# Router stage of a fused attention and expert kernel: TensorE filler work replaced, overflow inversion moved behind the transposes, second gather released earlier

## The chip, the cores and the metric

The kernel runs on one core of one Trainium2 chip. The metric is the device time of one execution in microseconds (us), lower is better. Three executions of the kernel before took 742.91, 743.01 and 746.74 us; the median is 743.01 us.

## The reference, cut to what matters

Three stages follow each other. All numbers are float32.

```python
# 1. attention with exponential gates: batch 2, 8 heads, 768 positions, head size 40
#    per position: decay state C and n, add v x k, y = sigmoid(o) * (C q) / max(|n q|, 1)
x = attn_out as rows                      # N = 1536 rows of 320

# 2. mixture of 8 experts, 320 -> 1024 -> 320, each row goes to its two best
noisy = x @ w_gate + log1p(exp(x @ w_noise)) * noise
top2  = two largest of noisy;  top2_w = softmax over the two
for e in range(8):
    for k in range(2):
        mask = top2[:, k] == e
        out[mask] += top2_w[mask, k, None] * (relu(x[mask] @ w1[e]) @ w2[e])

# 3. four experts, every row goes to all, weighted by normalised domain_probs
for e in range(4):
    out += p[:, e:e+1] * (relu(x @ w1b[e]) @ w2b[e])
```

## The kernel before, in words

The program is written out by hand, one instruction stream for each engine (`block.tensor`, `block.vector`, `block.scalar`, `block.gpsimd`, `block.sync`), and the streams meet only at semaphores (`wait_ge`). An engine works through its stream in order. Five stretches follow each other: attention (to about 90 us), the router (to about 124 us), the hand-over of the first tiles (to about 135 us), expert layer 1 (to about 361 us) and expert layer 2 (to the end). The change lies in the router's end and in the hand-over.

**Router.** DVE finds for each of the 24 pairs of choice and row tile (`2 * NT`) where its rows go. For every pair it writes `in_row` (L793) and `ids` (L794) and counts up `rt_place`. TensorE turns these lists round: 24 small bf16 matmuls (L1099), in six groups of four (`INV = 4`), accumulate into the bank `psI` (in the trace `psF`). DVE then writes the row numbers `rowid` (L798) and counts up `rt_rows`. With them GpSimd starts indirect DMAs (`gather`, L462): one fetches 128 rows of 320 numbers from DRAM into a part of `xrows`; four make one visit. The function `gather(v)` waits before visit 1 until the first hidden product of visit 0 is done (`h_mm[0]`), and from visit 2 on until the transposes of the visit that used the same buffer are done (`tr_mm[0]`).

**Filler.** `idle_work(n)` (L1091) issues n matmuls 128x512 whose result nobody reads. They stand in five places: three ahead of each group of the router's inversion but the first (15 in all), one each into two further banks and 16 more behind the last group, two ahead of tiles 1, 2 and 3 in the hand-over (6), and three at its end. All read the first weights of expert 0, which is why `wh_done[0]` is waited for ahead of them.

**Hand-over.** As each of the four tiles of visit 0 lands (`xin_first[tt]`), TensorE transposes it with four matmuls against the identity (L1109 to L1111), ScalarE copies the result rounded to fp32r (`x_hi`, L601, and `x_end`, L603), and DVE writes the rest (`x_lo`, L885, `x_end`, L887). Ahead of the filler and transposes of tile 3, TensorE waits for `over_picked` (set behind L831) and runs a second inversion of 24 small matmuls (L1192) into `psO` (in the trace `psL`) for the slots that hold an expert's overflow. DVE needs it at L890, once it has done tile 3's part, to make the row numbers of the overflow slots (`over_rows`) and the positions of results (`rt_dest`).

**Layer 1.** A loop of 8 visits, one expert and up to 512 rows each (`visit1`). TensorE reads two flags (`value_load`) and branches to a form of a visit with four tiles or with three (384 columns, taken by visit 0). A visit has 8 steps: `up` is eight matmuls into `pH` (L1132 to L1139), `down` is three matmuls a tile into `pY` (L1147 to L1149). Step s + 1's `up` is issued ahead of step s's `down`, which waits for DVE's `h_lo` (L848). During steps 4 to 6 the tiles of the next visit are transposed out of the other `xrows` buffer. SyncE loads the weights of the next expert as the pieces of the staging buffers come free.

Data products are split in a high and a low part, so each logical product is three matmuls.

## Time and profile before

| | |
|---|---|
| median of 3 runs | 743.01 us (742.91 to 746.74) |
| the profiled execution: its own time | 742.91 us |
| its span, first to last instruction | 741.0 us |
| mean granted TensorE clock | 0.972 of full |
| TensorE busy | 684.0 us (92%), 4064 matmuls |
| weight loads (beside the matmuls) | 612.5 us (83%) |
| DVE busy | 399.3 us (54%) |
| ScalarE busy | 287.0 us (39%) |
| GpSimd busy | 102.0 us (14%) |
| filler L1091 | 42 matmuls, 116.6 to 134.3 us |

Times in the rows are counted from the first instruction of the span. PE is TensorE's matmuls, PEld its weight loads, DVE VectorE, ACT ScalarE, POOL GpSimd, SP SyncE. The granted clock is a share of 2.4 GHz: 1.00 is 2.4 GHz and 0.50 is 1.2 GHz. A matmul's duration in the rows is its time through a pipeline; in a chain of them the distance between two starts is what one costs. The profiled execution's own time is 1.91 us longer than its span, and 0.10 us under the median.

### The profile page before, as it was taken

The numbers are of one execution on the slowest core, as the hardware profiler recorded it, in microseconds if no ns is written. First come the engines' busy times: TensorE is split into PE (matmuls) and PEld (weight loads), VectorE is DVE, ScalarE is ACT, GpSimd is POOL, SyncE is SP. The second block draws the span as 40 slices with busy tenths as digits, with TensorE's granted clock in tenths as the row PEclk, the third lists the DMA queues.
The fourth block names the chain that finished last, engine by engine and source line by source line (L and its number), as shares of the span: only waits on it lengthen the run. The fifth ranks groups of instructions, "written<-read, shape, count | busy, mean of one in ns | idle before, by whom it ended". The sixth has DMA issues, their size and how long they took to land.

```text
span 741.0 us, 11122 instructions
## 1 busy us (share of the span) xinstructions
PE 684.0 (92%) x4064; PEld 612.5 (83%) x4065; DVE 399.3 (54%) x667; ACT 287.0 (39%) x470; POOL 102.0 (14%) x137
## 2 busy tenths in 40 slices
PE   2999967899999999999469999999999999999997
PEld 2888824799889899899458998998898898988886
DVE  7667668656536456455155545545554554454422
ACT  6644530454434454454123324333343342332311
POOL 5343302431020220200140100201200001000000
PEclk9999887999999999999869999999999999999999
DMA  8566693375535455340175333343442333422000
GB/s 206 148 148 155 190 367 96 100 213 165 152 128 164 112 169 171 109 136 17 58 222 168 100 102 118 103 128 110 117 131 82 101 95 124 128 85 73 0 0 35
DMA packets 32566, 93.12 MB, mean 126 GB/s; under 512 B 4848, under 2 KB 14832, under 8 KB 32528
## 3 DMA queue, kind: packets, MB, share of 16 engines
q1 hardware_dynamic: 25040, 76.23, 35.5%
q0 software_dynamic: 3264, 11.15, 5.3%
q10 hardware_dynamic: 4224, 5.24, 1.9%
q8 instruction: 24, 0.39, 0.2%
q14 instruction: 14, 0.11, 0.1%
HBM read 79.49 MB, written 13.11 MB: 125 GB/s over the span
## 4 chain that ended last, share of the span: by engine, by line
PE 88%; DVE 5%; issue 2%; DMA 1%; POOL 1%; ACT 1%; DVEq 0%; ACTq 0%; POOLq 0%
PE pY L1147 12%; PE pY L1149 12%; PE pY L1148 12%; PE pH L1132 9%; PE pH L1133 9%; PE pH L1134 9%; PE pH L1139 5%; PE pH L1137 5%; PE psS L976 3%; PE psYa L1029 3%; PE pT L1109 2%; PE psYa L1042 1%; PE psF L1063 1%; PE pH L1091 1%; PE psD L986 1%
## 5 line engine op out<-in xcount | busy, mean ns | idle before, releaser
L576 ACT ACTIVATE h_hi<-pH 128x512 fp32r<-128x512 f32 x160 | 95.7, 598 | 290.1 <-PE pH L1139 290.1
L848 DVE SCALAR_TENSOR_TENSOR h_lo<-pH,h_hi 128x512 fp32r<-128x512 f32 x160 | 110.5, 691 | 174.1 <-ACT h_hi L576 173.0
L1147 PE MATMUL pY<-w_hi,h_hi 128*128 128x320 f32 x608 | 189.2, 311 | 3.9 <-DVE h_lo L848 3.3
L1149 PE MATMUL pY<-w_hi,h_lo 128*128 128x320 f32 x608 | 187.8, 309 | 0.0
L1148 PE MATMUL pY<-w_lo,h_hi 128*128 128x320 f32 x608 | 187.7, 309 | 0.0
L1132 PE MATMUL pH<-x_hi,w_hi 128*128 128x512 f32 (+2 forms) x324 | 126.9, 392 | 6.1 <-issue 3.6
L1147 PEld LDWEIGHTS pY<-w_hi,h_hi 128*128 128x128 f32 x608 | 114.2, 188 | 13.2 <-issue 6.5
L1133 PE MATMUL pH<-x_lo,w_hi 128*128 128x512 f32 (+2 forms) x324 | 123.7, 382 | 0.0
L1134 PE MATMUL pH<-x_hi,w_lo 128*128 128x512 f32 (+2 forms) x324 | 123.2, 380 | 0.0
L684 DVE TENSOR_TENSOR w_lo<-stage,w_hi 128x1024 fp32r<-128x1024 f32 (+1 forms) x79 | 107.1, 1357 | 25.5 <-ACT w_hi L522 25.4
L1148 PEld LDWEIGHTS pY<-w_lo,h_hi 128*128 128x128 f32 x608 | 114.2, 188 | 4.1
L1149 PEld LDWEIGHTS pY<-w_hi,h_lo 128*128 128x128 f32 x608 | 114.1, 188 | 0.0
L522 ACT ACTIVATE w_hi<-stage 128x1024 fp32r<-128x1024 f32 (+1 forms) x80 | 92.7, 1161 | 0.7 <-DMA stage<-in_w 0.7
L1132 PEld LDWEIGHTS pH<-x_hi,w_hi 128*128 128x128 f32 x324 | 61.4, 190 | 16.1 <-issue 8.3
L1134 PEld LDWEIGHTS pH<-x_hi,w_lo 128*128 128x128 f32 x324 | 61.3, 189 | 11.0
L1133 PEld LDWEIGHTS pH<-x_lo,w_hi 128*128 128x128 f32 x324 | 61.7, 190 | 6.0
L1139 PE MATMUL pH<-x_end,w_end 128*128 128x512 f32 (+2 forms) x162 | 61.3, 379 | 1.7 <-issue 1.7
L1137 PE MATMUL pH<-x_hi,w_end 128*128 128x512 f32 (+2 forms) x162 | 61.4, 379 | 0.0
L462 POOL DMA_INDIRECT xrows<-rows_by_token,rowid x36 | 36.2, 1007 | 175.1 <-PE pT L1111 126.6
L569 ACT ACTIVATE x_hi<-pT 128x512 fp32r<-128x512 f32 (+5 forms) x42 | 20.7, 504 | 59.7 <-PE pT L1109 35.7
L488 POOL DMA_INDIRECT G<-results_by_slot,dest x20 | 19.0, 951 | 164.3 <-DVE xrows L876 98.7
L1137 PEld LDWEIGHTS pH<-x_hi,w_end 128*128 128x128 f32 x162 | 30.6, 189 | 5.6
(222 smaller groups left out, 631.5 us busy)
## 6 DMA issues: line engine op xcount, KB each, us to landing
stage<-in_w SPq DMA_DIRECT2D x40, 640.0 KB, 3.9
stage<-in_w SPq DMA_DIRECT2D x40, 512.0 KB, 3.7
stage<-in_w SPq DMA_DIRECT2D x40, 256.0 KB, 3.9
results_by_slot<-acc ACTq DMA_DIRECT2D x8, 640.0 KB, 3.5
qk<-in_qk_t SPq DMA_DIRECT2D x16, 240.0 KB
kv<-in_kv_n SPq DMA_DIRECT2D x8, 480.0 KB
results_by_slot<-acc SPq DMA_DIRECT2D x6, 640.0 KB, 9.4
og<-in_o_n SPq DMA_DIRECT2D x2, 960.0 KB, 9.4
```

What stands on the lines that cost most here:

```text
L522: act.activation(hi, src, ACT.Copy).then_inc(wh_done[layer], 1)
L576: act.activation(HH[s % 2][:, :], pH[s % 2][:, :], ACT.Relu).then_inc(hh_done[layer], 1)
L684: dve.tensor_tensor(lo, src, f32(hi), ALU.subtract).then_inc(wl_done[layer], 1)
L848: dve.scalar_tensor_tensor(out=HL[s % 2][:, :], in0=pH[s % 2][:, :], scalar=0.0, in1=f32(HH[s % 2][:, :]), op0=ALU.max, op1=ALU.subtract). ...
L1132: pe.matmul(o, W1H[par][:, k, fs], XH[xpar][:, k, r], start=(k == 0), stop=False)
L1133: pe.matmul(o, W1H[par][:, k, fs], XL[xpar][:, k, r], start=False, stop=False)
L1134: pe.matmul(o, W1L[par][:, k, fs], XH[xpar][:, k, r], start=False, stop=False)
L1137: pe.matmul(o, W3[par][:, fs], XH[xpar][:, 2, r], start=False, stop=False)
L1139: ins = pe.matmul(o, W3[par][:, fs], XC[xpar][:, r], start=False, stop=True)
L1147: pe.matmul(y[:, 0:XD], hh, wh, start=(f == 0), stop=False)
L1148: pe.matmul(y[:, 0:XD], hh, wl, start=False, stop=False)
L1149: return pe.matmul(y[:, 0:XD], hl, wh, start=False, stop=(f == NF - 1))
```

## The change

Four things change, all in the router's end and the hand-over.

1. `idle_work` is gone with all its 42 matmuls (and the wait for `wh_done[0]`).
2. In its place stand seven matmuls behind the router's inversion. They wait for `rt_rows`, are bf16, 128x512, and read `iotaP` and `in_row`.
3. The overflow inversion (24 matmuls and the wait for `over_picked`) moves from ahead of tile 3's transposes to behind them.
4. `gather(1)` no longer waits for `h_mm[0]`.

```diff
@@ gpsimd, def gather(v)
-                if v == 1:
-                    pool.wait_ge(h_mm[0], 1)
-                elif v >= 2:
+                if v >= 2:
                     pool.wait_ge(tr_mm[0], 3 * (v - 2) + 6)
@@ tensor, router's end
-            def idle_work(n, bank=pH[0]):
-
-                for _ in range(n):
-                    pe.matmul(bank[:, :], W1H[0][:, 0, 0:P], W1H[0][:, 0, 0:512], start=True, stop=True)
-
-            pe.wait_ge(wh_done[0], 1)
             for n in range(2 * NT):
                 if n % INV == 0:
-                    if n >= INV:
-                        idle_work(3)
                     pe.wait_ge(rt_place, n + INV)
                 ins = pe.matmul(psI[:, 0:2 * MR], in_row[:, n, :], ids[:, n, :, :].rearrange("p n r -> p (n r)"), start=(n == 0), stop=(n == 2 * NT - 1))
             ins.then_inc(rt_inv, 1)
-            for bank in (pH[1], pY[3]):
-                idle_work(1, bank)
-            idle_work(16)
+            pe.wait_ge(rt_rows, 1)
+            keep_busy = in_row[:, 0:ST, :].rearrange("p n r -> p (n r)")
+            for bank in (*pH, pY[3], *pH, *pH):
+                pe.matmul(bank[:, :], iotaP[:, :], keep_busy, start=True, stop=True)
@@ tensor, hand-over
-                    if tt == ST - 1:
-                        pe.wait_ge(over_picked, 1)
-                        for m in range(2 * NT):
-                            ins = pe.matmul(psO[:, 0:2 * OVER * ST], in_row[:, m, :], over_ids[:, m, :, :].rearrange("p n r -> p (n r)"),
-                                            start=(m == 0), stop=(m == 2 * NT - 1))
-                        ins.then_inc(over_inv, 1)
-                    if tt > 0:
-                        idle_work(2)
                     pe.wait_ge(xin_first[tt], 16)
                     for k in range(3):
                         ins = turn(pF[half][k][:, n * P:(n + 1) * P], xrows[0][:, tt, :], k)
                         if n == 1:
                             ins.then_inc(tr_mm[0], 1)
-            idle_work(3)
+            pe.wait_ge(over_picked, 1)
+            for m in range(2 * NT):
+                ins = pe.matmul(psO[:, 0:2 * OVER * ST], in_row[:, m, :], over_ids[:, m, :, :].rearrange("p n r -> p (n r)"),
+                                start=(m == 0), stop=(m == 2 * NT - 1))
+            ins.then_inc(over_inv, 1)
             pe.wait_ge(rt_tiles, 1)
```

## Rows read from the trace of the kernel before

**Rows 1.** The page: shares of the chain that ended last, and granted clock by slice.
```profile
PE 88%; DVE 5%; issue 2%; DMA 1%; POOL 1%; ACT 1%; DVEq 0%; ACTq 0%; POOLq 0%
PEclk9999887999999999999869999999999999999999
```

**Rows 2.** Timeline of PE, router's end: start us, us for all, operation, x count, [idle before].
```profile
116.42 0.37 PE L1099 MATMUL psF<-ids,in_row 128*128 128x64 bf16 x4 [4.07 <-DVE ids L794]
...
123.62 0.29 PE L1099 MATMUL psF<-ids,in_row 128*128 128x64 bf16 x4
...
124.29 3.81 PE L1091 MATMUL pH<-w_hi 128*128 128x512 f32 x16
```

**Rows 3.** Timeline of DVE around the same waits: start us, us.
```profile
123.17 0.28 DVE L794 SCALAR_TENSOR_TENSOR ids<-row_of,hi,token 128x64 bf16<-128x64 f32 x1
...
129.99 0.51 DVE L831 TENSOR_SCALAR over_ids<-over_in,lane 128x576 bf16<-128x576 f32 x1
...
134.68 0.42 DVE L887 TENSOR_TENSOR x_end<-pH,x_hi 64x256 fp32r<-64x256 f32 x1 [0.18 <-ACT x_end L603]
...
135.75 0.18 DVE L890 COPY part<-psL 128x24 f32<-128x24 f32 x1
```

**Rows 4.** Timeline of POOL: gathers of visits 0 and 1.
```profile
124.67 1.18 POOL L462 DMA_INDIRECT xrows<-rows_by_token,rowid  x1 [30.91 <-DVE rowid L798]
...
128.70 1.40 POOL L462 DMA_INDIRECT xrows<-rows_by_token,rowid  x1 [0.30 <-issue]
139.20 0.94 POOL L462 DMA_INDIRECT xrows<-rows_by_token,rowid  x1 [9.10 <-PE pH L1139]
```

**Rows 5.** DMA: tile 3's gather, us to landing; instruction packets of 134 to 137.
```profile
xrows<-rows_by_token,rowid POOLq DMA_INDIRECT x1, 4.1
...
q8 instruction: 1, 0.02, 2.7%
```

**Rows 6.** Timeline of PE: overflow inversion, tile 3, last filler.
```profile
131.85 0.77 PE L1192 MATMUL psL<-over_ids,in_row 128*128 128x48 bf16 x24
...
133.02 0.38 PE L1109 MATMUL pY<-ident,xrows 128*128 128x128 f32 x2
...
133.37 0.94 PE L1091 MATMUL pH<-w_hi 128*128 128x512 f32 x3
```

**Rows 7.** Timeline of PE: the beginning of visit 0.
```profile
135.42 0.43 PE L1132 MATMUL pH<-x_hi,w_hi 128*128 128x384 f32 x1 [1.11 <-DVE x_end L887]
...
136.56 0.34 PE L1137 MATMUL pH<-x_hi,w_end 128*128 128x384 f32 x1
138.59 0.34 PE L1139 MATMUL pH<-x_end,w_end 128*128 128x384 f32 x1 [1.69 <-issue]
...
140.51 0.41 PE L1147 MATMUL pY<-w_hi,h_hi 128*128 128x320 f32 x1 [0.16 <-issue]
```

**Rows 8.** Windows where the clock rises: width, PE busy (count), clock, DMA share, GB/s.
```profile
91.00:92.00 1.00, 1.00 (x6) 0.74 1.01 364
...
122.00:122.25 0.25, 0.25 (x2) 0.52 0.00 0
...
381.50:382.00 0.50, 0.50 (x6) 0.85 1.00 385
```

**Rows 9.** Timeline of PE, elsewhere: work at the low clock, then at the full one.
```profile
87.36 2.77 PE L1072 MATMUL psTr<-ident,X 128*128 128x128 f32 x12
...
378.06 0.55 PE L1132 MATMUL pH<-x_hi,w_hi 128*128 128x256 f32 x1 [1.41 <-DVE x_end L844]
378.41 0.42 PE L1133 MATMUL pH<-x_lo,w_hi 128*128 128x256 f32 x1
378.62 0.41 PE L1134 MATMUL pH<-x_hi,w_lo 128*128 128x256 f32 x1
...
385.10 0.28 PE L1132 MATMUL pH<-x_hi,w_hi 128*128 128x256 f32 x1
385.21 0.28 PE L1133 MATMUL pH<-x_lo,w_hi 128*128 128x256 f32 x1
```

## The prediction, written before the change was run

> **What bounds the kernel now.** I read the page's chain first: 88% of it is TensorE, so a delay of TensorE in the hand-over or in layer 1 is a delay of the end, one for one [rows 1]. The slices beside it show the granted clock under full in only two regions, from 84 to about 122 us and around the change of layers [rows 1]. The change lies at the end of the first region and just behind it, and it can touch little else.
>
> Then the timelines. In the router's end DVE sets the pace. The last `ids` ends at 123.17 + 0.28 = 123.45 and the last group of four matmuls starts at 123.62 [rows 2, 3]. From there the path is `rowid`, the gathers from 124.67, tile 3's gather (issued 128.70, landed 4.1 later, at 132.80), its transposes at 133.02, DVE's last piece of it (134.68 + 0.42 = 135.10), and visit 0's first matmul at 135.42 [rows 3 to 7]. The filler fills the gaps ahead of these. The eighth matmul of visit 0 comes only at 138.59: 1.69 us of idle that the trace puts on issue, not on an engine, and the only DMA packet near it is one of instructions [rows 5, 7]. From 138.59 TensorE is dense.
>
> The clock: TensorE starts at 116.42, is never idle, and at 122.00 to 122.25 the clock turns from 0.50 (1.2 GHz) to full [rows 2, 8]. The rows behind it, visit 0 included, are at 2.4 GHz.
>
> **The change, part by part.**
>
> *Router's inversion without filler.* The first group ran at 1.2 GHz behind an idle engine and took 0.37; the last one, at 2.4 GHz, took 0.29 [rows 2]. Against DVE's `ids` the first group's lag is the same kind of latency (0.14 us or so behind the end of the fourth). I take 0.05 us later for `rt_rows`, with bounds 0 and 0.15 (all the 0.08 and a start 0.07 later).
>
> *Seven matmuls for eighteen.* They stand in the wait for tile 0's gather and delay nothing: at 1.2 GHz one takes about twice the 0.23 of the filler (3.81 for sixteen), so seven take about 3.2 us, from about 124.6 to 127.8, ahead of transposes at 129.6 [rows 2]. They are shorter than either stretch of work that was followed by a rise: 5.8 us from 116.42, and 3.6 us from 378.06 to about 381.65, where the stretch begun at 381.50 averages 0.85 [rows 2, 8, 9]. So I take the clock as still low when tile 0 lands. If it has risen, it is a rival.
>
> *Fillers ahead of tiles 1 to 3, and the overflow inversion out of the way.* In the kernel before, these lay beside the wait for the gather: tile 3 landed at 132.80 and its transposes began at 133.02 [rows 5, 6]. At most 0.22 us can be won. At 1.2 GHz a transpose costs about 0.23 (2.77 for twelve) [rows 9], so four tiles need about 0.9 each, still less than the 1.3 us between two gathers; only the first transpose of tile 3 is longer, by 0.1 to 0.2. Taken together +0.1 (bounds -0.2 and +0.3). ScalarE and DVE then need as long as before.
>
> *Overflow inversion behind tile 3.* Here is a cost. It took 0.77 us in a gap; now it stands between tile 3's transposes and visit 0's branch. Transposes at 132.9 to 133.8, then 24 small matmuls at 1.2 GHz, about 1.2 us (its 0.60 between starts, doubled), end at 135.0, where before the last filler ended at 133.37 + 0.94 = 134.31 [rows 6]. Before, 1.11 us passed from there to the first matmul. If this is the reading of the flags and the branch, visit 0 starts at 136.1, +0.7. If it was the wait for DVE's 135.10, nothing is lost, as that piece moves by 0.15 only. The first matmuls do not need that piece, so I take the former: +0.6 beyond the 0.15 of the terms above, bounds 0 and +1.2 (the inversion at 0.08 a matmul, as between the four of L1099 that took 0.37). DVE's L890, which waits for the inversion, was started at 135.75, later than 135.0, so its chain does not become the wait.
>
> *Visit 0 at 1.2 GHz.* A 256-column matmul costs 0.21 us at the low clock (378.41 to 378.62) and 0.117 at the full one (385.10 to 385.21) [rows 9]: of each low microsecond 0.45 is lost. The first seven matmuls cost nothing: at 384 columns they need some 0.32 each, 2.2 us, and the stall behind them, if it keeps its distance of 3.17 us from the first, covers that [rows 7]. So work resumes at 139.3. The clock rises 3.6 to 5.8 us of work after the start at 136.1, or, if the stall breaks that, after 139.3: between 139.7 and 145.1. I take 142.0, near the middle and equal to the longer stretch from the first start. Low from 139.3 to 142.0 loses 1.2 us, bounds 0.2 and 2.6. The wait at 140.51 (0.16, and the longer first step, 0.3 in all) disappears in the slower matmuls: 0.9 net, bounds 0 and 2.5.
>
> *`gather(1)` released at once.* GpSimd issues it from 130.1 instead of 139.20 [rows 4]. Nobody needs it before the transposes of visit 0's fourth step, about 150, and it was in time before. No gain. Its transfers now lie beside the end of tile 3's gather and the instruction packet; in the trace nothing else moves then [rows 5]. I take 0, bound +0.8 for both, since a gather alone took 4.1.
>
> Sum: 0.05 + 0.1 + 0.6 + 0.9 = 1.65 on the profiled execution's 742.91: 744.6 us. That execution is 0.10 under the median of 743.01, so 744.6 to 744.7; I give 744.6. By its bounds alone this case lies between 742.7 and 747.0.
>
> [...] Twelve transposes from 87.36 and little else precede the rise at 91.00 to 92.00 [rows 8, 9]. So the 16 transposes of the hand-over, with the small matmuls behind them some 5 us of nearly gapless work at 1.2 GHz, may bring the clock back by 133 to 135, ahead of visit 0. [...]
>
> **The rivals.**
>
> *The clock is back before visit 0.* For it: the row of transposes, and the seven matmuls. Against it: tile gaps, and a low clock that outlasts 2.4 us of filler from 116.42 [rows 2, 8]. Then 0.9 goes, and the inversion is partly quick: 742.91 + 0.15 + 0.4 = 743.5.
>
> *The fetch stall goes (the other side: faster).* The stall at the eighth matmul is tied to a place in TensorE's code, and 42 matmuls with their weight loads are taken out ahead of it and seven put in: 35 pairs fewer. If the place moves by these, the packet lands while other matmuls run, and 1.69 us at the full clock are won [rows 7]. With the inversion at +0.6 and +0.15 ahead of it, 742.91 - 1.69 + 0.75 = 742.0. It decides as soon as what the low clock costs in visit 0 is under 0.9. At the low clock throughout it gives only 743.4. [...]
>
> *The clock stays low long.* In the router it was low for 17 us, to 122.2. If visit 0's short waits hold it down for its first 11 us, that is 11 x 0.45 = 5 us: 748.0. Against it: every dense stretch in the trace has brought it up within 5.8 us.
>
> *Contention.* Gather 1 delays tile 3 and the instruction packet: forecast + 0.8, 745.4; inside the range.
>
> **How the numbers follow.** Forecast 0.42 (744.6). Clock back early 0.23 (743.5). Stall gone 0.17 (742.0, or 743.4 when the clock is low). Contention 0.08 (745.4). Low for long 0.07 (748.0). Something in layer 1 or 2 that the rows don't show 0.03. The range is 742.0 to 747.0. A measurement of this kernel can tell about 0.5% from no change, 3.7 us: faster than 739.3 asks for more than all stalls here together, 0.03; slower than 746.7 is the long low clock and the upper end of the forecast, 0.10; the rest, 0.87, is within.
>
> **What would show it.** The granted clock at 0.50 from 105 through 136 and its rise around 142; seven bf16 matmuls ending near 128; the overflow inversion behind 133.8 and the first matmul of visit 0 near 136.1, 1.1 behind its end; a stall of about 0.9 at the eighth matmul; four gathers from 130.1 on, with tile 3's landing unchanged; and visit 1 onward as before but later by under 2 us. A first matmul at 135.5 sinks the inversion's term; a full clock at 136 sinks the clock's; a gapless beginning of visit 0 is the rival of the stall. A difference over 4 us would mean that I looked at the wrong stretch.

## The result, and the profile after

The changed kernel took 746.91 us (median of 20 runs, 743.90 to 752.51), the kernel before, on the same chip, 742.66 us (20 runs, 740.37 to 746.74). The ratio is 1.0069 with an interval of 1.0053 to 1.0085: slower, by 4.3 us between the medians and by 5.1 us by the ratio. The forecast was +1.7 us on 742.91 and 0.87 for "no change that can be measured"; the case "slower" had 0.10. The median lies just inside the range, 742.0 to 747.0, but that is luck: the direction of the sum held, its size was a third to two fifths of what came, and, as the profile shows, most of it came from places to which the sum gave nothing.

The profiled execution of the changed kernel took 751.69 us, 4.8 above its median. Its page (the profile's first lines, the granted clock by slice, the chain's shares):

```profile
span 749.6 us, 11050 instructions
PE 677.4 (90%) x4028; PEld 606.8 (81%) x4030; DVE 399.5 (53%) x667; ACT 287.1 (38%) x470; POOL 100.6 (13%) x137
...
PEclk9999975699999999999969999999999999999999
...
PE 85%; DVE 6%; issue 3%; POOL 2%; DMA 1%; ACT 1%; another core or an unknown queue 1%; DVEq 0%; ACTq 0%; POOLq 0%
```

TensorE is busy for 6.6 us less and the span is 8.6 us longer. In the chain "issue" grew from 2% to 3%, and a releaser that the profile can't name has come in, "another core or an unknown queue" [rows 1]. The program runs on one core, so there is no other core to wait for: it is the first sign of what follows.

Where it happens, from the timeline of TensorE (start us, us for all, operation, count, [idle before]); this kernel's line numbers are 2 to 9 lower:

```profile
120.69 0.40 PE L1089 MATMUL psF<-ids,in_row 128*128 128x64 bf16 x4 [1.04 <-DVE ids L792]
122.00 0.63 PE L1094 MATMUL pH<-in_row,iotaP 128*128 128x512 bf16 x1 [0.91 <-DVE rowid L796]
...
122.85 1.91 PE L1094 MATMUL pH<-in_row,iotaP 128*128 128x512 bf16 x4
...
130.42 0.69 PE L1100 MATMUL pY<-ident,xrows 128*128 128x128 f32 x2 [1.30 <-DMA xrows<-rows_by_token,rowid]
...
131.12 0.42 PE L1102 MATMUL pH<-ident,xrows 128*64 128x128 f32 x1
131.33 1.17 PE L1187 MATMUL psL<-over_ids,in_row 128*128 128x48 bf16 x24
134.34 0.68 PE L1123 MATMUL pH<-x_hi,w_hi 128*128 128x384 f32 x1 [1.85 <-issue]
...
136.74 0.52 PE L1130 MATMUL pH<-x_end,w_end 128*128 128x384 f32 x1
...
139.30 0.52 PE L1130 MATMUL pH<-x_end,w_end 128*128 128x384 f32 x1
143.68 0.63 PE L1138 MATMUL pY<-w_hi,h_hi 128*128 128x320 f32 x1 [3.85 <-DVE h_lo L846]
...
168.97 0.43 PE L1123 MATMUL pH<-x_hi,w_hi 128*128 128x384 f32 x1 [2.43 <-issue]
```

The timelines of ScalarE, DVE and GpSimd for the same time:

```profile
130.93 0.66 ACT L599 ACTIVATE x_hi<-pY 128x256 fp32r<-128x256 f32 x2 [1.85 <-PE pY L1100]
...
139.33 0.60 ACT L574 ACTIVATE h_hi<-pH 128x512 fp32r<-128x512 f32 x1 [6.97 <-remote]
...
139.24 0.18 DVE L888 COPY part<-psL 128x24 f32<-128x24 f32 x1 [5.78 <-remote]
...
142.76 0.69 DVE L846 SCALAR_TENSOR_TENSOR h_lo<-pH,h_hi 128x512 fp32r<-128x512 f32 x1 [0.96 <-issue]
...
121.84 1.18 POOL L460 DMA_INDIRECT xrows<-rows_by_token,rowid  x1 [30.36 <-DVE rowid L796]
...
127.58 0.95 POOL L460 DMA_INDIRECT xrows<-rows_by_token,rowid  x1 [0.30 <-issue]
...
136.34 0.95 POOL L460 DMA_INDIRECT xrows<-rows_by_token,rowid  x1 [0.30 <-issue]
```

The clock, in windows (from:to, width, PE busy and count, clock, DMA share, GB/s):

```profile
126.00:132.00 6.00, 4.40 (x32) 0.50 0.50 122
...
134.00:138.00 4.00, 3.65 (x11) 0.50 0.50 136
140.00:141.00 1.00, 0.00 (x0) 0.88 0.00 0
144.00:147.00 3.00, 3.00 (x12) 0.50 0.40 98
147.00:148.00 1.00, 1.00 (x7) 0.96 0.99 295
```

The traces give the clock as a share of full speed; 2.4 GHz and 1.2 GHz in the prediction are its names for 1.00 and 0.50. An estimate of the speed behind them, from distances between starts: at 1.00 the matmuls of 384 columns in visit 0 are 0.174 us apart and the sixteen fillers of 512 0.228 (kernel before), 0.42 ns for each further column; at 0.50 those of 256 columns are 0.21 apart [rows 9] and the four of 512 from 122.85 on 0.427 (changed kernel), 0.85 ns for each.

**Counting.** The first gather stands at 121.84, before at 124.67 [rows 4]. The 2.83 us between them is attention, which the change doesn't touch; in two further profiles, one of each kernel, it stands at 124.23 and 124.13. So everything is counted from the first gather:

| event | before | after | difference |
|---|---|---|---|
| visit 0's first matmul | +10.75 | +12.50 | 1.75 |
| its 16th matmul starts | +15.35 | +17.46 | 2.11 |
| its first `down` matmul | +15.84 | +21.84 | 6.00 |
| the second step's `down` | +18.66 | +26.19 | 7.53 |
| visit 1's first `down` | +40.73 | +50.38 | 9.65 |
| layer 2's first transposes | +249.18 | +260.55 | 11.37 |

Then 0.1 more to the end: 11.43 - 2.83 = 8.6. Of the 11.4 us, five steps make 9.65: 1.75 ahead of visit 0; 0.4 in its first sixteen matmuls; 3.9 between the 16th and the first `down`; 1.5 behind it, in a second stretch at a granted clock of 0.50 (143.7 to 147.1); 2.1 up to visit 1's first `down`, as its first matmul waits 2.43 us on issue and did not wait before. The 1.69 us of [rows 7] at the eighth matmul are gone. The remaining 1.7 comes in small portions at later visits; two profiles of the kernel before differ by 1.1 at the same place (+249.18 and +250.24).

The 3.9 us: the eighth matmul, L1130, ends at 137.26, and ScalarE starts on its product at 139.33, 2.1 us later; before, the eighth ended at 138.93 and ScalarE started at 138.96. DVE's `part` waits for the inversion, over at 132.50, and starts at 139.24, 6.7 us behind it; before, DVE had other work until it was long done (132.62, and DVE at 135.75) [rows 3, 6]. Its chain of small steps then stands in front of `h_lo` until 141.80, so `down` starts at 143.68. Both engines woke within 0.1 us of each other, 2 us behind the end of GpSimd's last gather of a run of twelve (136.34 + 0.95 = 137.29). Not every signal in that run was late: at 130.93, during its eighth gather, ScalarE started on tile 3's first transposes as they ended.

This accounts for the 8.6 us of one pair of profiled executions. The medians differ by half of that, and the changed kernel's executions reach down to 743.90; which of these steps the quicker ones escape isn't shown, as only profiled executions have a trace.

### The profile page after: what moved, and what is told of

It is laid out like the page before. It is cut to its first block, busy times and chain, and to the rows that moved or that the text cites. A ratio compares the mean times of both kernels' runs of the same rounds, so it can differ in the third digit from the quotient of the medians.

```text
span 749.6 us, 11050 instructions
## 1 busy us (share of the span) xinstructions
PE 677.4 (90%) x4028; PEld 606.8 (81%) x4030; DVE 399.5 (53%) x667; ACT 287.1 (38%) x470; POOL 100.6 (13%) x137
## 4 chain that ended last, share of the span: by engine, by line
PE 85%; DVE 6%; issue 3%; POOL 2%; DMA 1%; ACT 1%; another core or an unknown queue 1%; DVEq 0%; ACTq 0%; POOLq 0%
PE pY L1138 12%; PE pY L1140 12%; PE pY L1139 12%; PE pH L1123 9%; PE pH L1124 9%; PE pH L1125 9%; PE pH L1130 4%; PE pH L1128 4%; PE psS L974 3%; PE psYa L1027 3%; PE pT L1100 1%; PE psYa L1040 1%; PE psF L1061 1%; DVE h_lo L846 1%; PE psD L984 1%
## 5 line engine op out<-in xcount | busy, mean ns | idle before, releaser
L1138 PEld LDWEIGHTS pY<-w_hi,h_hi 128*128 128x128 f32 x608 | 114.6, 188 | 18.2 <-issue 11.4
L1123 PEld LDWEIGHTS pH<-x_hi,w_hi 128*128 128x128 f32 x324 | 62.1, 192 | 17.7 <-issue 11.4
L1130 PE MATMUL pH<-x_end,w_end 128*128 128x512 f32 (+2 forms) x162 | 61.7, 381 | 0.0
```

The lines of the kernel that those rows point to most:

```text
L1123: pe.matmul(o, W1H[par][:, k, fs], XH[xpar][:, k, r], start=(k == 0), stop=False)
L1130: ins = pe.matmul(o, W3[par][:, fs], XC[xpar][:, r], start=False, stop=True)
L1138: pe.matmul(y[:, 0:XD], hh, wh, start=(f == 0), stop=False)
```

## The experiments

Ratios are to the kernel before in runs of the same series. Its median differed from series to series (743.49, 745.03, 743.54, 743.36), so medians of different series are not compared, and ratios of different series only roughly: the unaltered changed kernel has 1.0069 in one and 1.0105 in another. Where an experiment is one execution, it has no ratio. "+12.47" means 12.47 us behind the first gather.

**One part alone: `gather(1)` released.** Only the wait for `h_mm[0]` is taken away from the kernel before.

```diff
-                if v == 1:
-                    pool.wait_ge(h_mm[0], 1)
-                elif v >= 2:
+                if v >= 2:
```

> The kernel before, with one edit: gather(1) no longer waits for the first hidden product. Traffic theory (the gathers of visits 1 and 2, 12 us of transfers back to back, hold up something that DVE and ScalarE need at the start of layer 1, the 5.8 and 7.0 us waits of the changed kernel): 2 to 4 us slower than before, with the wait of DVE ahead of the second row-number copy seen again. Clock theory (all of the loss is TensorE at 1.2 GHz): within 0.5 us of before and no such wait. Code-place theory (fewer instructions ahead of the loop move the places where TensorE waits for code): as before, since no TensorE instruction changes.

Median 744.45, ratio 1.0013 (0.9987 to 1.0038). The median doesn't tell it from nothing; the profile shows visit 0 at +12.47 instead of +10.75, with ScalarE's first piece of tile 3 at 133.31 [4.29 <-remote], 1.1 us behind GpSimd's last issue (131.22 + 0.95), though its transposes (130.33 + 0.44) were there. Tile 0's and 1's transposes had reached ScalarE in time. GpSimd itself, idle since 132.17, saw the count of the transposes only at 133.62 [1.45 <-remote].

**One part alone: the inversion's place.** In the kernel before, the 24 matmuls move out of the loop over tiles. They stand behind the three last fillers; the expectation speaks of ahead of them.

```diff
-                    if tt == ST - 1:
-                        pe.wait_ge(over_picked, 1)
-                        (24 matmuls L1192)
             idle_work(3)
+            pe.wait_ge(over_picked, 1)
+            (24 matmuls L1192)
             pe.wait_ge(rt_tiles, 1)
```

> The kernel before, with one edit: the overflow inversion stands behind tile 3's transposes and ahead of the last three fillers. Traffic theory and clock theory: +0.2 to +0.8 us, the 0.6 us of 24 matmuls at the full clock on the path to visit 0. My prediction priced this term at +0.6. If the path to visit 0 is DVE's last piece of tile 3 instead: 0.

Median 748.59, ratio 1.0046 (1.0019 to 1.0073), far more than the +0.2 to +0.8 us expected, in two groups: three runs at 742.7 to 744.5, nine at 747.4 to 750.0. Timeline of TensorE, and windows of the clock:

```profile
133.34 0.78 PE L1199 MATMUL psL<-over_ids,in_row 128*128 128x48 bf16 x24
136.12 0.44 PE L1132 MATMUL pH<-x_hi,w_hi 128*128 128x384 f32 x1 [2.01 <-issue]
...
137.27 0.34 PE L1137 MATMUL pH<-x_hi,w_end 128*128 128x384 f32 x1
139.31 0.48 PE L1139 MATMUL pH<-x_end,w_end 128*128 128x384 f32 x1 [1.71 <-issue]
...
134.00:138.00 4.00, 1.60 (x12) 1.00 0.02 4
138.00:145.00 7.00, 5.69 (x20) 0.51 0.30 75
```

Even at a granted clock of 1.00 visit 0 is 1.35 us late (+12.10). The branch behind the fillers showed 1.11 us of idle; behind the 24 tiny matmuls 2.01. My estimate from these two gaps: with the reading of flags and the branch about 2.0 us pass to visit 0's first matmul, and three matmuls of 512 columns, still running meanwhile, cover 0.9 of it. That they run while TensorE reads flags isn't seen in any row. It isn't DVE: its last piece of tile 3 was done 1.83 us before visit 0's first matmul. And two gaps, 2.0 and 1.7, with seven matmuls between them, are followed by a fall to a granted clock of 0.50 for 6.8 us. In layer 1, ScalarE has a remote wait (3.71 us, to 151.58), for which TensorE waits 1.23 us.

**One part alone: the filler** (points 1 and 2 of the change: 42 matmuls out, seven in).

```diff
-            pe.wait_ge(wh_done[0], 1)
-            idle_work(...)            (15 + 2 + 16 + 6 + 3 matmuls)
+            pe.wait_ge(rt_rows, 1)
+            for bank in (*pH, pY[3], *pH, *pH):
+                pe.matmul(bank[:, :], iotaP[:, :], keep_busy, start=True, stop=True)
```

> The kernel before, with one edit: the 42 fillers are replaced by the seven bf16 matmuls. Clock theory: the clock is low into visit 0 and this alone gives most of the loss, +2 to +4 us. Code-place theory: in addition or instead a wait on issue of some 2.4 us at the start of visit 1, as in the changed kernel, +2 us even where the clock is full. Traffic theory: +0.5 to +1.5 us only, and no wait of 5 us on DVE.

Median 744.94, ratio 1.0020 (0.9996 to 1.0045). Visit 0 at +10.85, no wait at the eighth matmul, first `down` at +15.43. But at visit 1:

```profile
163.78 0.68 PE L1125 MATMUL pH<-x_hi,w_hi 128*128 128x384 f32 x1 [2.56 <-issue]
```

and the clock is low from 162.8 to 169.6; in visit 0 it is low from 135.4 to 138.9. One packet of instructions moved at 161.1, 2.7 us ahead of the end of that wait.

**The change with `gather(1)` gated again.**

```diff
-                if v >= 2:
+                if v == 1:
+                    pool.wait_ge(h_mm[0], 1)
+                elif v >= 2:
```

> The changed kernel, with one edit: gather(1) waits again for the first hidden product. Traffic theory: 2 to 4 us faster than the changed kernel, 743.5 to 745. Clock and code-place theories: as the changed kernel, 746 to 748, with the low clock in visit 0 and the wait on issue at visit 1.

Median 749.80, ratio 1.0066 (1.0033 to 1.0099), as the changed kernel. Visit 0 at +12.61, first `down` at +17.12 with nothing remote, visit 1 late by 2.68. It differs from the kernel of the filler alone only in the inversion's place: +1.76 us at visit 0's first matmul, +1.78 at TensorE's last wait of over 0.7 us, in layer 2 (507.24 and 505.46 behind the first gather). That is the inversion's price on the path in this pair, where 0.6 was forecast. Part of it is the clock: the inversion ran at a granted clock of 0.50 here (low until 138.0), while in the filler's kernel the clock was back at 132.1.

**The filler's work, at the same places in the code.** 39 of the 42 fillers get 48 columns instead of 512.

```diff
-                    pe.matmul(bank[:, :], W1H[0][:, 0, 0:P], W1H[0][:, 0, 0:512], start=True, stop=True)
+                    c = 48 if bank in written else 512
+                    written.append(bank)
+                    pe.matmul(bank[:, 0:c], W1H[0][:, 0, 0:P], W1H[0][:, 0, 0:c], start=True, stop=True)
```

> The kernel before, but 39 of its 42 fillers read 48 columns instead of 512 (the first into each of the three banks keeps 512). TensorE's stream has the same instructions at the same places; only the filler's work is gone. Clock theory: the clock stays at 1.2 GHz into visit 0 and this alone gives the loss of the kernel without fillers, +1.5 us (b_filler's median is 1.45 above before), the wait on issue stays at the eighth matmul of visit 0 and none of 2.5 us comes at visit 1. Code-place theory: the fillers' work is worth under 0.5 us, and b_filler's loss came from the wait at visit 1: within 0.7 us of before.

Median 745.56, ratio 0.9996 (0.9966 to 1.0025). What the filler does to the clock is worth nothing that can be measured, to within 0.3%. Windows of the clock:

```profile
130.00:131.00 1.00, 1.00 (x8) 0.50 0.05 15
131.00:132.00 1.00, 1.00 (x7) 0.50 0.53 118
132.00:133.00 1.00, 1.00 (x29) 0.87 0.11 31
135.00:136.00 1.00, 0.47 (x2) 0.84 0.08 16
136.00:139.00 3.00, 2.56 (x9) 0.50 0.00 0
```

The clock is back at 132.3, ahead of visit 0, and low again from 135.7 to 139.1. That costs little, because visit 0's slow first matmuls lie beside the wait on issue: at the eighth it is 0.44 instead of 1.69.

**The changed kernel with 35 pairs of weight load and matmul put back**, as matmuls of 48 columns behind the seven.

```diff
+            for _ in range(35):
+                pe.matmul(pH[0][:, 0:48], iotaP[:, :], in_row[:, 0, 0:48], start=True, stop=True)
```

> The changed kernel, with 35 small bf16 matmuls (48 columns) behind the seven, so that the code from there on stands as many instructions behind as before. Code-place theory: the wait on issue of 2.4 us ahead of visit 1's first matmul is gone, the one at the eighth matmul of visit 0 (1.7) is back, and as the second needs no relapse of the clock, 1 to 2.5 us faster than the changed kernel. If the wait at visit 1 has to do with the state of the buffers and not with where the code lies: it stays, and the time is the changed kernel's.

Median 746.36, ratio 1.0028 (1.0014 to 1.0042). The wait at visit 1 is gone, and at visit 0 there is one of 0.38 us, at the ninth matmul; so the place of the wait depends on the code ahead of it. What it is worth can't be read off here, as something else moved too: the run of gathers is eight long instead of twelve, and the first `down` stands at +18.43 instead of +21.84. Visit 0 is still at +12.40.

**The change with the inversion back ahead of tile 3, `gather(1)` free.**

```diff
+                    if tt == ST - 1:
+                        pe.wait_ge(over_picked, 1)
+                        (24 matmuls L1187)
                     pe.wait_ge(xin_first[tt], 16)
...
-            pe.wait_ge(over_picked, 1)
-            (24 matmuls L1187)
```

> The changed kernel, with the overflow inversion back ahead of tile 3's transposes. Theory of dispatch on the path (24 small matmuls between the last transpose and the branch cost about 1.5 us of issue, and the longer gap makes the clock fall back in some executions): 3 us faster than the changed kernel, first matmul of visit 0 about 10.8 us behind the first gather instead of 12.5, 744 to 745.5. Array theory (my prediction's 0.6 us): 0.6 us faster only, 746 to 747.

A miss: 751.69, ratio 1.0089 (1.0057 to 1.0121, six runs). Visit 0 stands at +12.55, but for another reason: ScalarE gets tile 3 at 139.75 [4.30 <-remote], 1.2 us behind GpSimd's last issue (138.51). Both faults act beside each other here, so taking one away gave nothing: the later one decides.

**Longer fillers in smaller number** (8 and 3 float32 ones for 16 and 6). They were meant to take eleven pairs out, and didn't: the trace shows each float32 one as two (the first eight are the x16 below, 0.43 us each at a granted clock of 1.00, so 0.87 for one filler where the old one cost 0.23; I had expected about twice).

```diff
+                    pe.matmul(pH[0][:, :], ident[:, :], X[:, :, :].rearrange("p t d -> p (t d)")[:, 0:512], start=True, stop=True)
...
-            idle_work(16)
+            long_work(8)
...
-                        idle_work(2)
+                        long_work(1)
```

> The kernel before, with 16 + 6 fillers replaced by 8 + 3 float32 fillers of the same width, which take about twice as long each: 11 pairs of instructions fewer at about the same filler work. Code-place theory: the wait on issue moves from the eighth matmul of visit 0 to about the 19th and shrinks, as by then 3 us have passed: under 0.5 us there; 0.5 to 1.5 us faster than before, unless a wait turns up at visit 1. Else: as before.

```profile
127.81 7.03 PE L1104 MATMUL pH<-X,ident 128*128 128x512 f32 x16
...
141.82 0.34 PE L1142 MATMUL pH<-x_hi,w_end 128*128 128x384 f32 x1
143.50 0.33 PE L1144 MATMUL pH<-x_end,w_end 128*128 128x384 f32 x1 [1.34 <-issue]
...
144.92 0.34 PE L1144 MATMUL pH<-x_end,w_end 128*128 128x384 f32 x1
```

Median 746.91, ratio 1.0018 (0.9997 to 1.0040). The profile has 4064 matmuls, as before, so no pair is missing, and the wait stays where it was, at the eighth matmul of visit 0 (143.50; the sixteenth is at 144.92). That agrees with a wait that hangs on the place of the code, but it doesn't test it. For the time it is confounded: the long fillers held up tile 0, and visit 0 came at +12.5.

**The inversion twice**, in the change with the gate, one execution.

```diff
+            for m in range(2 * NT):
+                pe.matmul(pH[0][:, 0:2 * OVER * ST], in_row[:, m, :], over_ids[:, m, :, :].rearrange("p n r -> p (n r)"), start=True, stop=True)
             (24 matmuls L1187 into psO)
```

> a_gate (the changed kernel with gather(1) waiting again) with the overflow inversion's 24 small matmuls issued twice behind tile 3, the first time into a bank nobody reads. Dispatch theory (about 0.06 us of issue for each small matmul with its weight load, once none is queued ahead): visit 0's first matmul 14.1 us or more behind the first gather, where a_gate had 12.61 and b_filler, with the inversion ahead of tile 3, 10.85: +1.5 to +1.8 for another 24. Array theory (0.05 us each at the low clock, 1.17 for the 24 in the changed kernel's trace): +1.2 at most. Branch theory (the difference came from the branch and not from the matmuls): no change.

Both sets ran at a granted clock of 1.00 (timeline of TensorE):

```profile
133.26 0.76 PE L1189 MATMUL pH<-over_ids,in_row 128*128 128x48 bf16 x24
133.87 0.76 PE L1192 MATMUL psL<-over_ids,in_row 128*128 128x48 bf16 x24
136.76 0.44 PE L1125 MATMUL pH<-x_hi,w_hi 128*128 128x384 f32 x1 [2.13 <-issue]
```

A set costs 0.61, the distance between the two starts, and the gap behind the last one stays at 2.1. So the price is no slow issue of the 24 matmuls; by the estimate above it is their time plus the cover that the branch has lost. Visit 0 is at +12.12. There is no wait for issue within visit 0, behind its first matmul, and none at visit 1, though 11 pairs are missing, and the clock doesn't fall: layer 2's first transposes stand at +251.05, where the kernel before has +249.18 and +250.24. So the inversion's new place alone is cheap where the clock and the wait on issue don't add to it.

**The gate alone, taken apart.** First: in the kernel before, `gather(1)` free and `gather(2)` held until the first hidden product, so that the run of indirect DMAs is eight long (one execution).

```diff
                 if v == 1:
+                    pass
+                elif v == 2:
+                    pool.wait_ge(tr_mm[0], 6)
                     pool.wait_ge(h_mm[0], 1)
-                elif v >= 2:
+                elif v > 2:
```

> The kernel before with gather(1) released at once but gather(2) waiting for the first hidden product. Theory that a gather under way holds back signals from TensorE to the other engines: a wait of DVE, ScalarE or GpSimd of 1 to 5 us is seen that ends behind 130 us of the trace although TensorE's matmul that it waits for is done, most likely at tile 3's transposes as in b_gather (4.3). Theory that it needs the eight gathers in a row: none.

Second: the same, with `gather(1)` as four plain DMAs of the same bytes (visit 1 then works on rows that aren't its own).

```diff
+                    if v == 1:
+                        pool.dma_start(xrows[1][:, tt, :], xd[(4 + tt) * P:(5 + tt) * P, :]).then_inc(xin[1], 16)
+                        continue
                     pool.indirect_dma_start(
```

> As d_first, but gather(1)'s four transfers are plain DMAs of consecutive rows (wrong rows for visit 1) issued by GpSimd, with the same bytes. Theory of traffic: the late signal is seen as in d_first. [...]

Timelines of the first, GpSimd, TensorE and ScalarE:

```profile
134.01 0.95 POOL L465 DMA_INDIRECT xrows<-rows_by_token,rowid  x1 [0.30 <-issue]
...
132.78 0.44 PE L1112 MATMUL pY<-ident,xrows 128*128 128x128 f32 x2
...
136.29 0.66 ACT L604 ACTIVATE x_hi<-pY 128x256 fp32r<-128x256 f32 x2 [4.60 <-remote]
```

and of the second, GpSimd and ScalarE:

```profile
130.21 2.23 POOL L466 DMA_DIRECT2D xrows<-rows_by_token  x4
...
133.85 0.66 ACT L607 ACTIVATE x_hi<-pY 128x256 fp32r<-128x256 f32 x2 [1.71 <-PE pY L1115]
```

The same transposes are seen by ScalarE 3.1 us behind their end with indirect DMAs (133.22 to 136.29), and at once with plain ones. Visit 0: +12.66 and +11.35. The bytes and the issuing engine are the same, so it isn't the amount of traffic. But the plain DMAs were issued in 2.23 us and over at 132.44, ahead of these transposes, while the indirect ones went on to 134.96. So whether it is indirect DMAs that delay signals, or any run of issues on GpSimd that is still going on, isn't separated.

**The filler's change with 21 pairs put back and nothing else**, the likeliest candidate for a better version.

```diff
+            for _ in range(21):
+                pe.matmul(pH[0][:, 0:48], iotaP[:, :], in_row[:, 0, 0:48], start=True, stop=True)
```

> A candidate for a better version: b_filler (seven matmuls for the 42 fillers, inversion ahead of tile 3, gather(1) waiting) with 21 small bf16 matmuls behind the seven, so that the code lies 14 pairs of instructions earlier than in the kernel before instead of 35. Code-place theory: the place of the wait is then some 14 matmuls further than the eighth of visit 0, by when the code is there, and the wait at visit 1 does not come: neither the 1.7 nor the 2.5 us, first down-matmul of visit 0 15 us behind the first gather instead of 15.8; 1 us faster than before, 2 to 3 faster than b_filler. If either wait is still there in full, the place theory lacks something.

Median 744.58, ratio 0.9998 (0.9976 to 1.0019): no better than before. The wait on issue didn't go, it stands at visit 0's first `down`, the seventeenth matmul:

```profile
140.75 0.41 PE L1142 MATMUL pY<-w_hi,h_hi 128*128 128x320 f32 x1 [2.45 <-issue]
```

With 14 pairs fewer it has moved by nine matmuls. No packet of instructions moved in the 5 us ahead of its end, unlike the other waits (see below), so that it is a wait for code is less sure here.

**Does it come each time?** Four kernels of one series: the changed one and the one before unaltered, the changed one with plain DMAs for `gather(1)` (and `gather(2)` held until the first hidden product), and the changed one with gate and 35 pairs, which keeps only the inversion's place and the cheaper filler.

> The changed kernel once more, unaltered. If late signals come in nearly every execution, this profile shows a remote wait of 1.5 us or more on ScalarE or DVE between the first gather and visit 0's first down matmul, which stands at +18 or later; if they are rare, it stands near +17.2 as in a_gate and nothing is remote. The wait for issue of 2.4 to 2.7 at visit 1's first matmul should be there again with the clock falling behind it. Ratio 1.006 to 1.008.

> The changed kernel, its gather(1) as four plain DMAs of the same bytes issued by GpSimd at the same place in its stream (visit 1 works on other rows; gather(2) waits for the first hidden product). Theory of late signals from indirect issue: no remote wait in the hand-over, visit 0's first down matmul near +17.2 as in a_gate instead of +21.8; the wait of 2.4 to 2.7 at visit 1 stays. Rival, traffic or the queue itself: remote waits of 2 us or more stay. If the late signals weigh in most executions, its ratio lies 0.3% or more under e_after2's; if they are rare, the two agree.

> The changed kernel with gather(1) gated again and the 35 matmul and weight-load pairs put back as 48-column matmuls ahead of the hand-over: of the change only the inversion's new place and the cheaper filler are left. If the price of the whole change is made of three parts (inversion's place, place of the wait for code, late signals), this one keeps the first alone: visit 0's first matmul 12.2 to 12.6 us behind the first gather, no wait for issue at visit 1, no remote wait ahead of 145 us; ratio 1.002 to 1.004. If the gate is worth nothing in most executions, it equals c_pad (1.0028). If the inversion's place costs nothing by itself, 1.000.

> The kernel before once more, unaltered. If the waits are tied to the program, the 1.7 us at the eighth matmul of visit 0 and the gap of 1.1 ahead of its first are there again, no clock falls between 122 and 370 us, and layer 2's first transposes start 249.2 us behind the first gather. If other gated kernels' late signals of layer 1 (148 to 151 us) are a matter of chance, they may show here: then 251 to 253.

The changed kernel: 752.87, ratio 1.0105 (1.0061 to 1.0149, six runs), more than expected. With plain DMAs: 748.11, 1.0064 (1.0033 to 1.0095). With gate and pairs: 744.84, 1.0014 (0.9986 to 1.0042). The first and the last of these intervals lie apart: gate and pairs together take back 0.9% in one and the same series. With both, visit 0 is at +11.60, earlier than the 12.2 to 12.6 expected, as the inversion ran at a granted clock of 1.00:

```profile
133.11 0.77 PE L1191 MATMUL psL<-over_ids,in_row 128*128 128x48 bf16 x24
135.88 0.68 PE L1127 MATMUL pH<-x_hi,w_hi 128*128 128x384 f32 x1 [2.00 <-issue]
```

The profile of the changed kernel repeats the late signals of the first one (timelines of ScalarE, DVE, GpSimd, TensorE):

```profile
141.40 0.60 ACT L574 ACTIVATE h_hi<-pH 128x512 fp32r<-128x512 f32 x1 [7.29 <-remote]
...
141.31 0.18 DVE L888 COPY part<-psL 128x24 f32<-128x24 f32 x1 [6.10 <-remote]
...
138.69 0.94 POOL L460 DMA_INDIRECT xrows<-rows_by_token,rowid  x1 [0.30 <-issue]
...
145.75 0.63 PE L1138 MATMUL pY<-w_hi,h_hi 128*128 128x320 f32 x1 [3.97 <-DVE h_lo L846]
```

First `down` at +21.52 (+21.84 the first time); with plain DMAs it is at +17.91 and nothing is remote. The second profile of the kernel before repeats its first: visit 0 at +10.75, `down` at +15.84, and the wait of [rows 7]:

```profile
138.04 0.34 PE L1139 MATMUL pH<-x_end,w_end 128*128 128x384 f32 x1 [1.68 <-issue]
```

It also had a remote wait of 2.82 us on ScalarE at 150.39, behind gathers from 138.65 to 149.9, where TensorE had other work; its only idle there, 0.27 us, is put down to the landing of a gather. So late signals come in the kernel before too, at a place with cover. They are no mishap of one execution.

## Why the prediction was wrong, step by step

**The bottleneck** (TensorE's path through the hand-over and layer 1) was read rightly: 9.65 of the 11.4 us arise there, up to visit 1's first `down`, and are still there at the end.

**`rt_rows` +0.05: right.** From the end of DVE's last `ids` to the first gather it is 1.22 us before (123.45 to 124.67) and 1.21 after (120.63 to 121.84). **Seven matmuls: right.** 2.8 us (122.00 to 124.76), over well ahead of tile 0.

**Tiles +0.1: too small, 0.6.** Tile 3's last transposition starts at +9.28 against +8.67, 0.2 of it from a later tile and the rest from the low clock.

**The inversion +0.6: the right mechanism, too small.** 1.76 us by the pair that differs in nothing else; over all profiles visit 0 starts at +11.60 to +12.78 with the inversion behind tile 3, and at +10.75 to +11.35 with it ahead, the kernels with late signals and with the longer fillers apart. What failed is the sentence on the 1.11 us of [rows 7]. I took it as the price of flags and branch and kept it. By my estimate from the gaps of 2.01 and 1.11 it was what is left of that price, about 2 us, behind matmuls that were still running: the three last fillers had paid 0.9 of it, and the inversion, ahead of tile 3, had cost nothing. The other reading that I had left open, a wait for DVE's last piece, is out: in six profiles visit 0 starts 0.3 to 0.9 us before that piece ends. The gap behind the 24 small matmuls was 1.7 to 2.2 us in six of eight profiles, and 2.6 and 2.9 in two (the second of the changed kernel, and the one with plain DMAs). Of the bounds, 0 to +1.2, the upper one was too low. In the kernel with gate and pairs, where the inversion ran at a granted clock of 1.00, visit 0 is only 0.85 us late.

**The clock, +0.9: 0.4 net in visit 0's first sixteen matmuls, and not tied to the filler.** In the changed kernel the clock stayed low to 140.2, and visit 0's sixteen matmuls took 4.96 us from first start to last instead of 4.60: +0.4 net. But it isn't tied to the filler. With fillers of 48 columns the clock was back at 132.3, with the filler's change alone at 132.1, and in the second profile of the changed kernel at 131.6. In the last one the router's small matmuls, the seven, and twelve transposes (128.3 to 131.1) precede it. So my rival "the clock is back before visit 0" came true there, and yet the clock fell again behind the branch's gap. Whether transposes bring the clock up isn't settled: in these three profiles a rise stands behind transposes, and in the first profile of the changed kernel the same instructions brought none before 140.2. My own row for it was thin as well: ahead of the twelve transposes at 87.36 TensorE had been dense with small matmuls since 79.8, and six more transposes ran from 90.39 up to the rise. The ratio of the kernel with short fillers, 0.9996, says that the filler's work at this place buys nothing that can be measured.

**The stall of the fetch: half right.** The rival said that the place moves with the 35 pairs and that 1.7 us are won. It moved, from visit 0's eighth matmul to visit 1's first, where nothing covers it, so the -1.69 didn't show: 2.2 to 2.7 us in all six profiles of kernels with the 35 pairs out, and in four of them a stretch at a granted clock of 0.50 of 3.4 to 6.8 us with it. My sum had no term for visit 1. Putting the pairs back with the gate takes the ratio from 1.0066 to 1.0014, across two series and with intervals that overlap, and layer 2's first transposes from +256.18 to +252.26. That it is code that is waited for is my reading and rests on the DMA view alone: the only packet of instructions near each of these waits moves 2.3 to 3.2 us ahead of its end, at visit 0's eighth matmul (135.8, wait to 138.59) as at visit 1's first (166.2, wait to 168.97). The rule "the place moves by the pairs" isn't borne out as a count: 14 pairs fewer moved it by nine matmuls, and with 11 fewer, in the kernel with two inversions, there is no wait at all. All these waits stand at or close behind a branch: at visit 1's first matmul (2.2 to 2.7 us), or at the eighth (0.3 to 1.7), the ninth (0.3 to 0.4) or the seventeenth (2.45) of visit 0.

**`gather(1)` at 0, bound +0.8: wrong, and for a cost that I didn't have.** I weighed its transfers and tile 3's landing. The landing is unchanged (its transposes 4.55 us behind its issue, before 4.32). What came late were the signals: while GpSimd issues indirect DMAs back to back, some counts raised by TensorE reach ScalarE and DVE only 1 to 2 us behind the end of the run. In six of six profiles with `gather(1)` free and indirect it happened in the hand-over or in visit 0's first step; in five of them it cost 1.7 us or more on the path, in the one with 35 pairs put back about 0.9 (first `down` at +18.43, with the gate at +17.58). The gate on `h_mm[0]` put the next four gathers behind the hand-over. In the median, though, its removal alone isn't told from nothing (1.0013).

**The sum.** Its bounds were added up wrongly: the upper ones give 742.91 + 0.15 + 0.3 + 1.2 + 2.5 = 747.1, and 747.9 with the gather's 0.8, not 747.0. What the parts cost, by ratios: inversion's place and cheap filler, 1.0014; with the gather free 1.0028; with the code shifted as well 1.0069. Or from single parts: filler with its shifted code 0.20%, inversion's place 0.46%, gather 0.13%, together 0.79%, against 0.69 measured. The filler's and the gather's part lie within the resolution of a comparison, so this division is rough, and no part can be named the largest. In microseconds of the one profile: 1.75 (0.75 forecast), 0.4 (0.9), late signals 3.9 (0), second low stretch 1.5 (0), visit 1 2.1 (-0 to -1.7).

**What stays open.** The late signals cost about 4 us in both profiles of the changed kernel, and 0.4% between its form with indirect and with plain DMAs, but the two intervals overlap, and the gated form has the same ratio as the free one in another series (1.0066 and 1.0069). The inversion's place costs 0.46% alone and, with gate and pairs, at most 0.42%: how much it costs depends on whether the clock falls behind the gap, and what decides that I can't say. Why signals come late is not seen in any row, nor why others in the same run come in time, nor whether it is the indirect DMAs or any long run of issues. No version was faster than the kernel before.

## What to carry to other kernels

An idle of 1.1 us ahead of a branch may not be the branch's price but what running matmuls left of it; here it was 1.7 to 2.9 us behind small ones. Before shortening the last work ahead of a loop, ask what the idle would be without it, and keep wide matmuls there. Instructions have a place as well as a time; taking 35 pairs out moved a wait on issue to another instruction, one with no cover (from visit 0's eighth matmul, 1.7 us, to visit 1's first, 2.2 to 2.7). A gate that seems to guard only a buffer may also keep a burst of indirect DMAs away from a chain of signals (with it visit 0's first `down` stood at +17.12, without it at +21.84). Before removing it, look at what the other engines hand each other in the time that the burst will take.

## What the runs showed of the hardware

- Signals from TensorE to ScalarE and DVE came late beside indirect DMAs on GpSimd: 4.3 to 4.6 us of remote wait with eight in a row, 7.0 and 7.3 with twelve; 1.0 in the kernel with 35 pairs put back, with eight; none in the hand-over with four indirect and four plain ones, or with four alone. In the five profiles with 4.3 us or more the wait ends 1.1 to 2.0 us behind the last issue. Others end within a run: in the kernel with 35 pairs put back ScalarE's first signal of tile 0 (129.91), in the one with short fillers one in layer 1 (148.10). GpSimd's own waits for TensorE's count were late too, by 1.4 to 1.6 us, in three profiles.
- A wait on issue on TensorE that goes with a packet of instructions moved 2.3 to 3.2 us ahead of its end: 0.3 to 2.7 us, at one instruction, the same in both profiles of each of the two kernels profiled twice. It was at the eighth or ninth matmul of visit 0 where as many pairs stood ahead of it as before, and elsewhere, or absent, where fewer did.
- Between the last small matmul ahead of visit 0's branch and visit 0's first matmul TensorE was idle for 1.7 to 2.9 us in eight profiles; behind three matmuls of 512 columns for 1.1 to 1.3 us in three, and for 0.12 in the kernel with longer fillers.
- The granted clock fell from 1.00 to 0.50 behind many gaps of 2 us or more ahead of visit 0 or visit 1, and stayed there for 3.4 or 6.8 us, but not behind all: at visit 1 in four of six profiles, and not behind the 2.13 us of the kernel with two inversions. With short fillers it fell behind 1.52 us. The gaps of 1.1 and 1.7 us in the kernel before (1.25 and 1.68 in its second profile) didn't bring it down.
